# The flags of the search spread from 128 rows instead of 8

## The chip, the core and the metric

The kernel runs on one core of a Trainium2 chip (trn2). The metric is device time in microseconds for one execution of the whole program, the median over several runs. The engines are TensorE (PE in the rows, its weight loads PEld), VectorE (DVE), ScalarE (ACT), GpSimd (POOL) and SyncE (SP, which issues DMAs). They run side by side and wait for each other by semaphores.

## What is computed

Three parts follow each other: a gated linear attention over 4 x 8 heads of 768 steps, an assignment of 3072 tokens to 8 experts with room for exactly 384 tokens each, whose two matrices are then applied, and a gated two-branch layer at the end.

```python
def _moe_ref(x, w_gate, w1, w2):
    cap = N // E                       # 384
    logits = x @ w_gate
    order = np.argsort(-logits.flatten())
    for idx in order:                  # best (token, expert) pair first
        tok, e = int(idx) // E, int(idx) % E
        if assigned[tok] >= 0 or counts[e] >= cap:
            continue
        assigned[tok] = e
        counts[e] += 1
    for e in range(E):
        h = np.maximum(x[assigned == e] @ w1[e], 0.0)
        out[assigned == e] = h @ w2[e]

def _moe2_ref(x, w_a, w_b, w_out):
    return (x @ w_a) * (x @ w_b) @ w_out
```

The greedy order is what makes the assignment hard: which token an expert takes depends on which experts are already full.

## The kernel before

The first stage (attention, the block of lines 167 to 633) leaves the logits in SBUF, token by token on 128 partitions and 24 tiles. The second stage (experts) does the rest in eight turns, one for each expert in the order in which they fill up. It has one instruction stream for each engine, written out by hand; the order within a stream is the order of execution, and semaphores tie the streams together.

**A turn.** TensorE computes, for the 384 tokens of one expert, eight upward tiles (`up`, 8 products of 128x128 by 128x384 each), eight downward tiles (`down`, 9 products), then twelve pairs of the second layer (`pair`, 2 x 8 products into psA and psB) and twelve projections (`project`, 9 products of 320 columns). Each value is split into a high and a low part, which is why there are three products where one would do. In the rows the upward products and the pairs all have line 897, the downward ones line 920, the projections line 947. ACT copies and rounds what comes out, VectorE makes the low parts and the product of a and b (lines 1376, 1380).

**The search.** While turn k runs, the same engines look for the expert that is full next and for its tokens, in the first six turns (a first search, before turn 0, has nothing beside it). A search is a number search in ROUNDS = 11 rounds, each of which fixes one digit. One round is a relay:

1. VectorE, `compare` (line 1156): which keys reach each of 15 or 16 thresholds, into cmp.
2. TensorE, `count` (line 959), three products of the flags with the proposals, into psG; in the first search `count_tiles` (line 967) instead.
3. VectorE, `tally` (lines 1199, 1202), then TensorE, `gather_counts` (line 973), 8 rows by 16 sums into psN16.
4. VectorE, `is_full` (line 1206): for each expert and threshold, is the count at the limit; the answers, 0 or the step of the digit, go to the tile `full` (8 partitions, 15 columns, bfloat16).
5. TensorE, `spread` (line 978): ones times full, so that each of the 128 partitions gets, for each threshold, the sum over the eight experts, into psF.
6. VectorE, `narrow` (line 1214, any_full): the sum becomes the next base; then the next compare.

**Where a round stands in a turn.** For rounds 0 to 5 the spread stands in the middle of an upward tile, behind its third product. Round 6 has no upward tile left and its spread stands alone between `gather_counts` and `down`. Round 7 stands within the psB half of pair 0. Rounds 8, 9 and 10 stand behind projections 0, 1 and 2. Behind projection 3 TensorE does `total` (line 982): the tile of ones, 128 x 128, times mine, 128 x 8, with a wait of its own on VectorE.

GpSimd makes the constant tiles at the end of the first stage (lines 294 to 307), and VectorE waits for all of them at line 613.

Of the kernel before, what the change touches and what calls it, by code (L numbers as in the profile page):

```python
# [7 lines left out]
ALU = mybir.AluOpType  # L8
# [3 lines left out]
F32R = mybir.dt.float32r  # L12
BF16 = mybir.dt.bfloat16
# [3 lines left out]
P = 128  # L17
B, H, S, D = 4, 8, 768, 40
E = 8
DM = H * D  # L20
NT = B * S
CAP = NT // E
# [32 lines left out]
def build(nc, qk, tok, ig, fg, w_gate, w1, w2, w_a, w_b, w_out, out, xs, parts):  # L55
    with ExitStack() as ctx:
        logit = ctx.enter_context(nc.sbuf_tensor("logit", [P, TILES, E], F32))
        identf = ctx.enter_context(nc.sbuf_tensor("identf", [P, P], F32))

        wa = ctx.enter_context(nc.sbuf_tensor("wa", [P, 5, F2], F32R))  # L60
        wb = ctx.enter_context(nc.sbuf_tensor("wb", [P, 5, F2], F32R))
        second = (wa, wb)
        fixed = search_tensors(nc, ctx)
        with ExitStack() as inner:
            attention(nc, inner, logit, identf, qk, tok, ig, fg, w_gate, xs, parts, fixed)
        with ExitStack() as inner:
            experts(nc, inner, logit, identf, second, w_a, w_b, w_out, w1, w2, xs, out, fixed)


def search_tensors(nc, ctx):  # L70
    def sb(name, shape, dt=F32):
        return ctx.enter_context(nc.sbuf_tensor(name, shape, dt))

    return {
        "rown": sb("rown", [P, TILES]), "tilev": sb("tilev", [P, TILES]), "pv": sb("pv", [P, 1]), "digit": sb("digit", [P, 16]),
        "slot": sb("slot", [P, P], BF16), "tie8": sb("tie8", [P, E]), "cols": sb("cols", [P, CAP // P]),
        "ones": sb("ones", [P, P], BF16), "onward": sb("onward", [P, P], BF16),
        "run_on": sb("run_on", [P, TILES]),
        "steps_of": sb("steps_of", [P, len(STEPS), 16]), "start_at": sb("start_at", [P, 3]),
        "sel": sb("sel", [P, TILES]), "was_full": sb("was_full", [P, E]),  # L80
        "own": sb("own", [GI, GJ]), "fold": sb("fold", [GI, 16], F32R),
    }


def attention(nc, ctx, logit, identf, qk, tok, ig, fg, w_gate, xs, parts, fixed):
# [6 lines left out]
    def sem(name):  # L92
        return ctx.enter_context(nc.semaphore(name))
# [68 lines left out]
    sm = {n: sem(n) for n in names}  # L162
# [60 lines left out]
    def _(pool):  # L223
# [77 lines left out]
        pool.memset(fixed["ones"][:, :], 1.0).then_inc(sm["made"], 1)  # L301
        pool.memset(fixed["run_on"][:, :], 1.0).then_inc(sm["made"], 1)
        pool.iota(place_i, [[-16, GJ], [-1, 16]], base=0, channel_multiplier=1).then_inc(sm["made"], 1)
        pool.wait_ge(sm["made"], 10)

        pool.affine_select(out=fixed["onward"][:, :], in_=fixed["ones"][:, :], compare_op=ALU.is_ge, fill=0.0, base=0,
                           pattern=[[-1, P]], channel_multiplier=1).then_inc(sm["made"], 1)
# [168 lines left out]
    def _(dve):  # L476
# [133 lines left out]

        ct = Count(dve, sm["cast_done"])
        also, step = ct.also, ct.step
        dve.wait_ge(sm["made"], 11)
        also(dve.tensor_copy(fixed["rown"][:, :], rowi))
        also(dve.tensor_copy(fixed["tilev"][:, :], tilei))
        also(dve.tensor_copy(fixed["pv"][:, :], pi))
# [19 lines left out]
class Count:  # L636
# [8 lines left out]
    def also(self, ins):  # L645

        self.n += 1
        ins.then_inc(self.sem, 1)
# [11 lines left out]
DIGITS = [(lv, s, i == 0, i == len(digits) - 1) for lv, digits in enumerate(SEARCHES) for i, s in enumerate(digits)]  # L660
# [9 lines left out]
GJ = TILES // NG  # L670
GI = GJ * 16


def experts(nc, ctx, logit, identf, second, w_a, w_b, w_out, w1, w2, xs, out, fixed):
# [8 lines left out]
    def sb(name, shape, dt=F32):  # L683
        return ctx.enter_context(nc.sbuf_tensor(name, shape, dt))
# [4 lines left out]
    def sem(name):  # L689
        return ctx.enter_context(nc.semaphore(name))  # L690
# [41 lines left out]
    rown, tilev, pv, slot, tie8, cols, ones = (fixed[n] for n in """rown tilev pv slot tie8 cols ones""".split())  # L732
    onward, run_on, steps_of, start_at, sel, was_full, own, fold = (fixed[n] for n in """onward run_on steps_of start_at sel was_full own fold""".split())
# [14 lines left out]
    eq = sb("eq", [P, TILES])  # L748
    base = [sb(f"base{n}", [P, 1]) for n in range(2)]
    cmp = sb("cmp", [P, TILES, 16], BF16)  # L750
    full = sb("full", [E, 15], BF16)
    own_cnt = sb("own_cnt", [GI, E, GJ])
    part_cnt = sb("part_cnt", [GI, E], F32R)
    any_full = sb("any_full", [P, 15])
# [31 lines left out]
    psN = psT[:, at:at + 15]  # L786
    psN16 = psT[:, at:at + 16]
    psG = psT[0:GI, 0:GJ * E]
    psF = psT[:, at + 16:at + 31]
# [9 lines left out]
    sm = {n: sem(n) for n in names}  # L799
# [79 lines left out]
    def _(pe):  # L879
# [95 lines left out]
        def spread(p, r):  # L975

            pe.wait_ge(sm["full_ready"], p * ROUNDS + r + 1)
            pe.matmul(psF, ones[0:E, :], full[:, :], start=True, stop=True).then_inc(sm["spread"], 1)  # L978

        def total(p):  # L980
            pe.wait_ge(sm["given_ready"], p + 1)
# [16 lines left out]
        with pe.Fori(0, ROUNDS) as r:  # L998
            count_tiles(r)
            spread(0, r)  # L1000
# [10 lines left out]
        def turn(k, beside):  # L1011
            p = k + 1
            search = beside == "search"
            for f in range(FT):
                if f < FT - 1:
                    up(k, f + 1, (lambda: spread(p, f - 1)) if search and f else None)
                elif search:
                    spread(p, f - 1)
                down(k, f, (lambda: count(p, f)) if search else None)
                if search:  # L1020
                    gather_counts(p, f)
# [125 lines left out]
    def _(dve):  # L1147
# [55 lines left out]

        def is_full(p, r):
            dve.wait_ge(sm["counted"], p * ROUNDS + r + 1)
            dve.tensor_scalar(full[:, :], psN[0:E, :], CAP - 0.5, float(DIGITS[r][1]), ALU.is_ge, ALU.mult
                              ).then_inc(sm["full_ready"], 1)

        def narrow(p, r):
# [129 lines left out]
        start = ct.n  # L1339
        for r in range(ROUNDS):  # L1340
            is_full(0, r)
            narrow(0, r)
# [23 lines left out]
        def turn(k, beside):  # L1366
# [17 lines left out]
            for f in range(FT - 1):  # L1384
                if search and f:
                    narrow(p, f - 1)
                if search:
                    tally(p, f)
                h_low(k, f + 1)
                if search:  # L1390
                    is_full(p, f)
                if early and f in SPLIT_EARLY:
                    low_parts(0, SPLIT_EARLY[f])
                if early and f == WO_EARLY:
                    low_out(0)
# [6 lines left out]
            if search:  # L1402
                is_full(p, FT - 1)
                narrow(p, FT - 1)
# [89 lines left out]
```

## Time and profile before

| | us |
|---|---|
| median of 3 runs | 919.02 |
| lowest and highest run | 914.65, 921.96 |
| profiled execution | 922.04 |
| its span, first to last instruction | 920.3 |
| TensorE matmul busy | 812.3 (88%) |
| VectorE busy | 609.3 (66%) |
| ScalarE busy | 287.1 (31%) |
| GpSimd busy | 169.8 (18%) |

The busy time of TensorE is that of its products with their modelled ends; products follow each other more closely than they last, so the distance from start to start says more than the duration of one. A row of the timeline gives the start, the duration, the engine, the line and the tiles that are written and read; behind it, in brackets, how long the engine was idle before and who released it.

### The profile page before, as it was taken

Reading aid. Unit: us, or ns where it says so; the run is one execution under the profiler, and the core shown is the slowest. Engines: PE = TensorE matmul, PEld = TensorE weight load, DVE = VectorE, ACT = ScalarE, POOL = GpSimd, SP = SyncE. Lnnn points to the kernel's source line nnn. Section 1 sums busy time; section 2 is a strip of 40 time slices with the busy share of each in tenths; the row PEclk is TensorE's granted clock in tenths of the full one; section 3 lists DMA queues with packets and bytes.
Section 4 is the critical chain, followed back from the end, with each engine's and each line's share of the span. In section 5 each row is a group of like instructions: output and inputs, shape, how many; then the busy total and the mean of one; then the engine's idle time right before and its main releaser. Section 6 shows DMA issues by size and latency. Waiting matters only on the chain.

```text
span 920.3 us, 16627 instructions
## 1 busy us (share of the span) xinstructions
PE 812.3 (88%) x5858; PEld 752.0 (82%) x5858; DVE 609.3 (66%) x1756; ACT 287.1 (31%) x538; POOL 169.8 (18%) x195
## 2 busy tenths in 40 slices
PE   1999999322789999999999999999999999999995
PEld 0899999211669988998898889889978999999995
DVE  7778888667557876686668567856876683374221
ACT  4434442211223432252234123412432252243221
POOL 6555665281000110011002001100110011011001
PEclk9999999555789999999999999999999999999998
DMA  4866661603200410130023003200500230050000
GB/s 115 246 190 209 208 207 61 213 0 116 75 22 22 134 37 2 47 102 21 0 63 92 15 0 97 71 0 2 141 25 0 63 84 22 1 137 34 1 1 22
DMA packets 51624, 66.63 MB, mean 72 GB/s; under 512 B 6376, under 2 KB 42232, under 8 KB 51576
## 3 DMA queue, kind: packets, MB, share of 16 engines
q1 hardware_dynamic: 37352, 50.31, 18.0%
q0 software_dynamic: 2368, 7.88, 3.1%
q10 hardware_dynamic: 11856, 7.87, 2.8%
q8 instruction: 22, 0.36, 0.2%
q14 instruction: 26, 0.21, 0.1%
HBM read 57.88 MB, written 8.16 MB: 72 GB/s over the span
## 4 chain that ended last, share of the span: by engine, by line
PE 50%; DVE 23%; issue 3%; ACT 3%; DMA 1%; POOL 1%; SPq 0%; DVEq 0%; ACTq 0%; POOLq 0%
PE psA L897 21%; PE acc L920 11%; PE psB L897 8%; PE acc L947 7%; DVE at_slot L1294 3%; DVE ab L1376 2%; DVE ab_lo L1380 2%; DVE w_lo L1318 2%; ACT ab_hi L1120 2%; DVE cmp L1156 2%; DVE w_lo L1314 2%; PE psT L978 1%; DVE w_hi L1316 1%; PE psT L959 1%; PE psT L967 1%
## 5 line engine op out<-in xcount | busy, mean ns | idle before, releaser
L897 PE MATMUL psA<-x_hi,wa 128*128 128x384 f32 x480 | 136.2, 348 | 0.5 <-DVE x_lo L1401 0.4
L897 PE MATMUL psB<-x_hi,wb 128*128 128x384 f32 x480 | 131.8, 339 | 0.0
L852 POOL DMA_INDIRECT xg<-xs_dram,idx_g x24 | 25.1, 1046 | 468.0 <-DVE idx_g L1308 463.2
L1129 ACT COPY a_sb<-psA 128x384 f32<-128x384 f32 x96 | 46.1, 480 | 174.9 <-PE psB L897 174.9
L897 PE MATMUL psA<-x_lo,wa 128*128 128x384 f32 x288 | 96.8, 336 | 0.0
L897 PE MATMUL psB<-x_lo,wb 128*128 128x384 f32 x288 | 96.5, 335 | 0.0
L947 PE MATMUL acc<-wo_hi,ab_hi 128*128 128x320 f32 x288 | 92.9, 323 | 1.0 <-DVE ab_lo L1380 1.0
L1376 DVE TENSOR_TENSOR ab<-a_sb,psB 128x384 f32<-128x384 f32 x96 | 52.9, 551 | 58.4 <-ACT a_sb L1129 57.4
L947 PE MATMUL acc<-wo_lo,ab_hi 128*128 128x320 f32 x288 | 88.9, 309 | 0.0
L947 PE MATMUL acc<-wo_hi,ab_lo 128*128 128x320 f32 x288 | 88.8, 308 | 0.0
L1380 DVE TENSOR_TENSOR ab_lo<-ab,ab_hi 128x384 fp32r<-128x384 f32 x96 | 53.6, 559 | 52.3 <-ACT ab_hi L1120 48.1
L897 PE MATMUL psA<-x_hi,w_hi 128*128 128x384 f32 x192 | 74.6, 388 | 14.3 <-DVE w_lo L1321 7.5
L897 PEld LDWEIGHTS psA<-x_hi,wa 128*128 128x128 f32 x480 | 83.1, 188 | 4.1 <-DVE x_lo L1401 2.1
L897 PEld LDWEIGHTS psB<-x_hi,wb 128*128 128x128 f32 x480 | 85.9, 188 | 0.1
L1104 ACT ACTIVATE h_hi<-psA 128x384 fp32r<-128x384 f32 x64 | 31.5, 492 | 173.5 <-PE psA L897 168.5
L1120 ACT CAST ab_hi<-ab 128x384 fp32r<-128x384 f32 x96 | 49.2, 513 | 92.2 <-DVE ab L1376 92.2
L920 PE MATMUL acc<-h_hi,w_hi 128*128 128x384 f32 x192 | 71.1, 371 | 0.0
L897 PE MATMUL psA<-x_lo,w_hi 128*128 128x384 f32 x192 | 66.3, 345 | 0.0
L920 PE MATMUL acc<-h_lo,w_hi 128*128 128x384 f32 x192 | 65.9, 343 | 0.0
L920 PE MATMUL acc<-h_hi,w_lo 128*128 128x384 f32 x192 | 65.7, 342 | 0.0
L874 POOL DMA_INDIRECT out_dram<-o_sb,idx_s x24 | 24.1, 1003 | 190.1 <-ACT o_sb L1084 185.2
L947 PEld LDWEIGHTS acc<-wo_hi,ab_hi 128*128 128x128 f32 x288 | 54.1, 188 | 3.9 <-DVE ab_lo L1380 3.1
(236 smaller groups left out, 1742.9 us busy)
## 6 DMA issues: line engine op xcount, KB each, us to landing
w_raw<-in_w_dram SPq DMA_DIRECT2D x32, 320.0 KB, 3.1
w_raw<-in_w_dram SPq DMA_DIRECT2D x32, 256.0 KB, 3.0
toks<-in_tok_dram SPq DMA_DIRECT2D x24, 324.0 KB, 3.6
qks<-in_qk_dram SPq DMA_DIRECT2D x48, 160.0 KB
w_raw<-in_w_dram SPq DMA_DIRECT2D x64, 64.0 KB, 2.8
gate<-in_tok_dram SPq DMA_DIRECT2D x6, 640.0 KB, 5.7
xs_dram<-y ACTq DMA_DIRECT2D x24, 160.0 KB, 3.4
qst<-in_qk_dram ACTq DMA_DIRECT2D x48, 60.0 KB
```

What stands on the lines that cost most here:

```text
L852: pool.indirect_dma_start(out=xg[:, t, 0:DM], out_offset=None, in_=xrows, in_offset=bass.IndirectOffsetOnAxis(ap=idx_g[:, t:t + 1], axis=0 ...
L874: pool.indirect_dma_start(out=out, out_offset=bass.IndirectOffsetOnAxis(ap=idx_s[:, t:t + 1], axis=0), in_=o_sb[:, t, :], in_offset=None). ...
L897: last = pe.matmul(ps, w, x, start=(n == 0), stop=(n == len(steps) - 1))
L920: last = pe.matmul(acc[m][:, 0:CAP], w[q][:, f % FQ, c], x[n][:, :], start=(f == 0 and j == 0), stop=(f == FT - 1 and j == 2))
L947: last = pe.matmul(acc[t][:, 0:DM], x[n][:, c], w[:, g, :], start=(g == 0 and j == 0), stop=(g == GT - 1 and j == 2))
L1104: act.activation(h_hi[f % 2][:, :], psA[f % 2][:, 0:CAP], ACT.Relu).then_inc(sm["h_hi_ready"], 1)
L1120: act.copy(ab_hi[g % 2][:, :], ab[g % 2][:, :]).then_inc(sm["ab_hi_ready"], 1)
L1129: act.copy(a_sb[g % 2][:, :], psA[g % 2][:, 0:CAP]).then_inc(sm["a_copied"], 1)
L1156: dve.scalar_tensor_tensor(out=cmp[:, :, :], in0=key[lv][:, :].unsqueeze(2).broadcast_to([P, TILES, 16]), scalar=start_at[:, lv:lv + 1] if ...
L1294: last = dve.tensor_scalar(at_slot[i][:, j, :], slot[:, :], prow[:, i * ST + j:i * ST + j + 1], None, ALU.is_equal)
L1376: dve.tensor_tensor(ab[g % 2][:, :], a_sb[g % 2][:, :], psB[g % 2][:, 0:CAP], ALU.mult).then_inc(sm["ab_done"], 1)
L1380: dve.tensor_tensor(ab_lo[g % 2][:, :], ab[g % 2][:, :], f32(ab_hi[g % 2][:, :]), ALU.subtract).then_inc(sm["ab_ready"], 1)
```

## The change

The tile `full` gets 128 partitions in place of 8. It moves from the second stage's own tiles to those that live through both stages. GpSimd sets it to zero once, near the end of the first stage, and counts that on the semaphore `made`, whose two waits ask for one more. `is_full` writes the first eight partitions, as before. `spread` now multiplies the whole 128 x 128 tile of ones by all 128 rows of `full`; rows 8 to 127 are zero, so the sums are the same.

```diff
@@ search_tensors
-        "own": sb("own", [GI, GJ]), "fold": sb("fold", [GI, 16], F32R),
+        "full": sb("full", [P, 15], BF16), "own": sb("own", [GI, GJ]), "fold": sb("fold", [GI, 16], F32R),
@@ attention, GpSimd
-        pool.wait_ge(sm["made"], 10)
+        pool.memset(fixed["full"][:, :], 0.0).then_inc(sm["made"], 1)
+        pool.wait_ge(sm["made"], 11)
@@ attention, VectorE
-        dve.wait_ge(sm["made"], 11)
+        dve.wait_ge(sm["made"], 12)
@@ experts
-    full = sb("full", [E, 15], BF16)
+    full = fixed["full"]
@@ experts, TensorE, spread
-            pe.matmul(psF, ones[0:E, :], full[:, :], start=True, stop=True).then_inc(sm["spread"], 1)
+            pe.matmul(psF, ones[:, :], full[:, :], start=True, stop=True).then_inc(sm["spread"], 1)
@@ experts, VectorE, is_full
-            dve.tensor_scalar(full[:, :], psN[0:E, :], CAP - 0.5, float(DIGITS[r][1]), ALU.is_ge, ALU.mult
+            dve.tensor_scalar(full[0:E, :], psN[0:E, :], CAP - 0.5, float(DIGITS[r][1]), ALU.is_ge, ALU.mult
```

On GpSimd, at the end of the first stage, the program before (the names are tiles, the numbers partitions by elements):

```order
L301 MEMSET ones 128x128
L302 MEMSET run_on 128x24
L303 IOTA ints 128x128
L306 AFFINE_SELECT onward<-ones 128x128
L64 UNCONDITIONAL_BRANCH
```

and the changed one:

```order
L301 MEMSET ones 128x128
L302 MEMSET run_on 128x24
L303 IOTA ints 128x128
L304 MEMSET full 128x15
L307 AFFINE_SELECT onward<-ones 128x128
L64 UNCONDITIONAL_BRANCH
```

One memset has come in ahead of the last constant; on TensorE, VectorE, ScalarE and SyncE the instructions and their order are the same, only that `spread` reads 128 rows. The tiles that are allocated behind `full` in its new place all start 32 bytes later in their partitions.

## Rows read from the trace of the kernel before

**Rows 1.** The page: TensorE's granted clock, in tenths, over 40 slices.
```profile
PEclk9999999555789999999999999999999999999998
```

**Rows 2.** Line 978, TensorE's idle time before it: releaser, us, times.
```profile
  issue: 14.2, 60
```

**Rows 3.** The chain of waits: start us, us, what; one turn and the next.
```profile
414.18 1.65 PE psA L897 x8
...
463.68 0.11 PE psT L978
...
471.05 0.49 ACT a_sb L1129
...
500.24 1.65 PE psA L897 x8
```

**Rows 4.** Timeline, TensorE, a spread behind a projection: start us, us, engine, line, operation.
```profile
626.02 0.31 PE L947 MATMUL acc<-wo_hi,ab_lo 128*128 128x320 f32 x1
626.26 0.18 PE L978 MATMUL psT<-full,ones 8*128 8x15 bf16 x1
626.37 0.62 PE L897 MATMUL psA<-x_hi,wa 128*128 128x384 f32 x2
626.82 0.34 PE L897 MATMUL psA<-x_lo,wa 128*128 128x384 f32 x1
```

**Rows 5.** Timeline, TensorE, the total behind projection 3 of the same turn.
```profile
639.86 0.31 PE L947 MATMUL acc<-wo_hi,ab_lo 128*128 128x320 f32 x1
640.01 0.18 PE L982 MATMUL psT<-mine,ones 128*128 128x8 bf16 x1
640.05 0.60 PE L897 MATMUL psA<-x_hi,wa 128*128 128x384 f32 x2
640.48 0.35 PE L897 MATMUL psA<-x_lo,wa 128*128 128x384 f32 x1
```

**Rows 6.** Timeline, TensorE, round 0: the spread in an upward tile, and the count after.
```profile
422.23 0.34 PE L897 MATMUL psA<-x_lo,w_hi 128*128 128x384 f32 x1
422.50 0.18 PE L978 MATMUL psT<-full,ones 8*128 8x15 bf16 x1
422.61 0.44 PE L897 MATMUL psA<-x_hi,w_hi 128*128 128x384 f32 x1
422.89 0.34 PE L897 MATMUL psA<-x_hi,w_lo 128*128 128x384 f32 x1
423.06 0.34 PE L897 MATMUL psA<-x_lo,w_hi 128*128 128x384 f32 x1
...
424.11 0.26 PE L959 MATMUL psT<-ohc,cmp 128*128 128x64 bf16 x3
```

**Rows 7.** Timeline, VectorE, the compares behind the spreads of rounds 0 and 3.
```profile
422.99 0.62 DVE L1156 SCALAR_TENSOR_TENSOR cmp<-key,base,steps_of 128x384 bf16<-128x384 f32 x1
...
434.25 0.62 DVE L1156 SCALAR_TENSOR_TENSOR cmp<-key,start_at,steps_of 128x384 bf16<-128x384 f32 x1
```

**Rows 8.** Timeline, TensorE, the count behind the spread of round 3.
```profile
434.62 0.34 PE L920 MATMUL acc<-h_lo,w_hi 128*128 128x384 f32 x1
434.92 0.26 PE L959 MATMUL psT<-ohc,cmp 128*128 128x64 bf16 x3
```

**Rows 9.** Timeline, TensorE, the count behind the spread of round 6.
```profile
444.90 0.26 PE L959 MATMUL psT<-ohc,cmp 128*128 128x64 bf16 x3 [0.27 <-DVE cmp L1156]
```

**Rows 10.** Timeline, VectorE, first search: reads of a spread's and of the total's result.
```profile
171.89 0.23 DVE L1214 TENSOR_SCALAR_CACHE_REDUCE any_full<-psT,start_at 128x15 f32<-128x15 f32 x1 [0.28 <-PE psT L978]
...
208.83 0.17 DVE L1246 TENSOR_SCALAR now_full<-psT 128x8 f32<-128x8 f32 x1 [0.28 <-PE psT L982]
```

**Rows 11.** Timeline, the end of the first stage: GpSimd's constants, VectorE's first use.
```profile
162.05 0.47 POOL L306 TENSOR_SCALAR_AFFINE_SELECT onward<-ones 128x128 bf16<-128x128 bf16 x1
...
162.88 0.17 DVE L614 CAST rown<-ints 128x24 f32<-128x24 int32 x1
```

**Rows 12.** Line 286: engine, operation, count; duration ns min/median/max, first and last start.
```profile
L286 POOL TENSOR_TENSOR st_old<-state,dec x24: 727/737/744, 25.6 to 156.0; 120x328 f32<-120x328 f32 x24
```

## The prediction

> **What bounds the kernel now.** I read the page first, for the clock: TensorE is granted its higher level, 2.4 GHz, but for the first search and the start of the first turn [rows 1]. The profiled execution took 922.04 us, 1.7 us more than its span of 920.3 and 3.0 us above the median of 919.02. Then the line of the matmul that the change touches, line 978. It runs 7 x 11 = 77 times, 66 of them inside the six turns that carry a search, and before 60 of them TensorE's array stood without a new start for 14.2 us in all, 0.24 us each, with no engine named as the releaser [rows 2]. Then the chain of waits, to see whether TensorE's time counts there. In a steady turn (the same row comes back after 86.06 us) the chain lies on TensorE for most of the way from the first upward product at 414.18 to the end of pair 5 at 471.05, where ACT takes it over, and the last spread, at 463.68, is on it [rows 3]. From there it runs over VectorE (places, one-hot tiles, weight splits) for 29.2 us, until the next turn's first product at 500.24. The spreads all lie in the TensorE part. So a spread that costs less shortens the turn, as long as VectorE's part of the round doesn't come last.
>
> **What a spread costs now.** I read it from start to start in TensorE's timeline. Behind a projection [rows 4]: from the last product of the projection to the spread 0.24, to the next pair 0.11, to its third product 0.45: 0.80 us. The closest thing to the changed spread is already in the program, in the same place behind a later projection: the total of line 982, the same 128x128 tile of ones against 8 columns from all 128 rows, with a semaphore wait of the same kind in front of it [rows 5]: 0.15, 0.04 and 0.43, so 0.62 us. The two differ by 0.18. Without either matmul it would be 0.15 and two times 0.17 (the pitch, below), about 0.50: the spread costs 0.30, the total 0.12. In the middle of an upward product [rows 6]: 0.27, 0.11, 0.28, against a pitch of 0.17 between undisturbed products (422.89 to 423.06), so 0.66 in place of 0.35, a cost of 0.31; with the total's 0.12 in its place the saving is 0.19. What the rows show is a wait of about 0.1 us ahead of the 8-row matmul and another 0.1 behind it, which the 128-row one in the same place doesn't have. That the number of rows is the cause is what I infer: output partitions, stationary tile, type and wait are the same in both.
>
> **Which of the eleven rounds give it back.** Rounds 0, 1, 2, 4 and 5 stand in upward tiles with room behind them: VectorE's compare of round 0 ends at 423.61, the count that needs it starts at 424.11 [rows 6, 7]. They give 5 x 0.19 = 0.95. Round 3 has two more VectorE steps (eq, key), and its successor already waits: the count starts 0.30 after the product in front of it, not 0.17, and cmp ended 0.05 before it [rows 7, 8]. Only the part ahead of the spread counts there, 0.27 - 0.17 = 0.10; the part behind it turns into a longer wait for cmp. Round 6 has no products between its sums and its spread, so the spread starts when VectorE has written full, and the count behind it waits another 0.27 us for cmp [rows 9]: whatever TensorE saves there it waits. So it gives nothing. Round 7, in the psB half of the first pair, stands among products of the same 384 columns as an upward tile's and has a count far behind it: 0.19. Rounds 8, 9 and 10 follow projections: 3 x 0.18 = 0.54. That makes 0.95 + 0.10 + 0 + 0.19 + 0.54 = 1.78 us a turn, times six turns 10.7 us. In the first of them two spreads run at or near 1.2 GHz [rows 1]; I take the same 0.19 for them, since a wait at the lower clock can only be as long or longer in time. The bounds of this sum: from below 6 x 10 x 0.07 = 4.2 us, if only the gap behind the spread goes (0.11 against 0.04) and the wait ahead of it belongs to the semaphore; from above 6 x 11 x 0.31 = 20 us, the whole cost of a spread as if it took nothing. I take the value of the total because its row is the same operation in the same place.
>
> **The other edits.** In the first search every round is a serial relay of TensorE and VectorE. From the end of VectorE's write to its next read of the result the trace shows 0.28 us of idle around the 8-row spread and 0.28 around the total there [rows 10]. So 128 rows cost and save nothing in these eleven: 0, give or take 11 x 0.01. VectorE writes 8 rows of full as before. The memset is one more GpSimd instruction in front of affine_select; a memset of 15 columns can hardly take longer than that affine_select over 128 columns, 0.47 us, which ends at 162.52, while VectorE, whose wait now asks for one more, starts on the constants only at 162.88 [rows 11]. The cover is 0.36 us, so I take 0; at 0.47 it would be 0.11 once. The new place of full moves every tile allocated behind it by its 30 bytes, rounded up; that is a rival below. The sum is -10.7 us: 922.04 gives 911.4 for an execution like the profiled one, and from the median 919.02 it gives 908.3. I predict 908.5.
>
> **What the skill says against it.** The 8-row spread lasts 0.18 us and the 128-row total 0.18 [rows 4, 5], so by durations alone nothing is won. The Trainium skill ("TensorE: Matmul & The Clock Gate", section "Why this matters for your kernels") says that a single matmul with a contraction of 32 takes as long as one with 128, and gains only where several run side by side. By that the sum would be zero and the time 919. The durations agree with it; the starts in the same rows don't, and my sum goes by the starts.
>
> **Rivals.**
> 1. The forecast, chance 0.73.
> 2. Part of it is lost on VectorE (0.11). After a spread VectorE does any_full and cmp and is done 1.11 us after the spread's start, while TensorE has 1.61 us of products before the count [rows 6, 7]. The change takes about 0.09 off TensorE's side, and 0.05 goes from the end of cmp to the count [rows 7, 8]. That leaves 0.3 to 0.4 us, so I expect no wait; if the arrival of cmp mattered in all rounds as in round 3, each of the ten would give 0.10, so 1.0 us a turn, 6 us in all: 913.
> 3. Nothing changes (0.09). The idle time ahead of line 978 would be the price of its wait on a semaphore, with the weights fetched only after it. For it: the profile names no releaser. Against: the total waits too and shows no gap [rows 5]. Time 919.
> 4. Slower (0.03). The 32-byte step moves the operands of the turns (all but wa and wb, which are allocated ahead of it) from a multiple of 64 bytes to an odd multiple of 32. If TensorE read them more slowly there, the place would be each of the 436 large products of a turn; about two thirds of them lie on the chain, 2,300 over eight turns. The gain is gone at 10.7 / 2,300 = 4.6 ns per product, and 1% slower, 928, needs (10.7 + 9.2) / 2,300 = 8.7 ns on a pitch of 0.17 us [rows 6]. Against: in the first stage buffers whose size is an odd multiple of 32 bytes (st_old, 1312 bytes) stand at both kinds of address in turn, and over all of them GpSimd's durations spread by 17 ns in 737 [rows 12]. That is another engine, so it weighs less than it seems.
> 5. More than forecast, 12 to 15 us (0.04), if the waits at the lower clock are dearer or a shorter first turn brings the full clock earlier: 905.
>
> **Range and chances.** The forecast's own range is 906 to 912: 9 to 12 us off a base that itself ran from 914.65 to 921.96. The 80% range takes in most of the partial case and the rival with more: 904 to 914.5; outside it lie no change, slower, and the tails. A change of 1% (9.2 us) is about what a measurement of this kernel can tell from no change, and the forecast stands only 1.5 us beyond it. I give faster by over 1% 0.68 (most of the forecast, and the fifth case), within 1% 0.29 (the rest of the forecast, the partial case and no change), slower 0.03.
>
> **What the changed profile would show.** Line 979 in place of 978, 128 rows, with its idle time by issue gone from 14.2 us to a few; starts of 0.15, 0.04, 0.43 around a spread behind a projection and about 0.17, 0.04, 0.26 in an upward tile; the wait in front of the count of round 3 up from 0.12 to about 0.2; round 6 as before; turns of 84.3 us in place of 86.06; the stretch in which VectorE leads unchanged at 29 us; the first search as long as before. I am wrong if the intervals stay at 0.27 and 0.11 (rival 3), if they shrink but the turn doesn't (rival 2), or if the pitch of 0.17 between products grows (rival 4).

## The result and the profile after

| | before | changed |
|---|---|---|
| median of 11 runs, us | 918.89 | 912.33 |
| lowest and highest run | 914.65, 921.96 | 906.65, 914.73 |
| profiled execution | 922.04 | 909.61 |
| its span | 920.3 | 907.9 |

The ratio of the changed kernel to the one before is 0.9926 (95% interval 0.9905 to 0.9946): 6.8 us less (5.0 to 8.7), where 10.7 were worked out and 908.5 us predicted. The time lies in the 80% range (904 to 914.5), but just above the forecast's own 906 to 912, and the gain is a third short. It is a change of 0.7%; the prediction had given 0.68 to more than 1% and 0.29 to less. The two profiled executions are 12.4 us apart and would hide the missing third, so part of the question is what they leave out.

**The spread.** All of the changed kernel's lines have moved up by one; line 979 is the spread. The view of that line, its idle time and who waited for it:

```profile
L979 PE MATMUL psT<-full,ones x77: 182/183/237, 171.2 to 708.9; 128*128 128x15 bf16 x77
its engine sat idle before it (us, times) until:
  DVE full L1207: 11.8, 34
  issue: 6.8, 42
```

The idle time that no engine was named for has fallen from 14.2 us in 60 places [rows 2] to 6.8 in 42; what is behind VectorE's full stays at 11.8. The timeline of TensorE in the changed kernel, round 0 of the same turn, in an upward tile (start us, us, engine, line, operation):

```profile
415.88 0.33 PE L921 MATMUL acc<-h_lo,w_hi 128*128 128x384 f32 x1
416.05 0.17 PE L974 MATMUL psT<-fold,part_cnt 128*8 128x16 f32 x1
416.08 0.42 PE L898 MATMUL psA<-x_hi,w_hi 128*128 128x384 f32 x1
416.34 0.34 PE L898 MATMUL psA<-x_hi,w_lo 128*128 128x384 f32 x1
416.51 0.34 PE L898 MATMUL psA<-x_lo,w_hi 128*128 128x384 f32 x1
416.69 0.18 PE L979 MATMUL psT<-full,ones 128*128 128x15 bf16 x1
416.73 0.42 PE L898 MATMUL psA<-x_hi,w_hi 128*128 128x384 f32 x1
416.99 0.34 PE L898 MATMUL psA<-x_hi,w_lo 128*128 128x384 f32 x1
```

Around the spread, from start to start, this is 0.18, 0.04 and 0.26 us, against 0.27, 0.11 and 0.28 [rows 6]: 0.18 less. The same view behind a projection, and the total further on:

```profile
446.98 0.31 PE L948 MATMUL acc<-wo_hi,ab_lo 128*128 128x320 f32 x1
447.13 0.18 PE L979 MATMUL psT<-full,ones 128*128 128x15 bf16 x1
447.17 0.59 PE L898 MATMUL psA<-x_hi,wa 128*128 128x384 f32 x2
447.60 0.34 PE L898 MATMUL psA<-x_lo,wa 128*128 128x384 f32 x1
...
460.45 0.18 PE L983 MATMUL psT<-mine,ones 128*128 128x8 bf16 x1
...
544.68 0.18 PE L983 MATMUL psT<-mine,ones 128*128 128x8 bf16 x1
```

0.15, 0.04 and 0.43: the spread now has exactly the intervals of the total [rows 5], where it had 0.24, 0.11 and 0.45 [rows 4]. The last two rows are a turn apart: 84.23 us, and the five such distances of this execution are 84.16 to 84.27, where it was 86.06 [rows 3] (85.94 to 86.06 over all five). That is 1.8 us a turn; the forecast had 1.78.

**The two rounds that were to give less.** The same view at the count of round 3 and around the spread of round 6:

```profile
428.17 0.34 PE L921 MATMUL acc<-h_lo,w_hi 128*128 128x384 f32 x1
428.57 0.26 PE L960 MATMUL psT<-ohc,cmp 128*128 128x64 bf16 x3
...
436.55 0.17 PE L974 MATMUL psT<-fold,part_cnt 128*8 128x16 f32 x1
437.01 0.18 PE L979 MATMUL psT<-full,ones 128*128 128x15 bf16 x1 [0.28 <-DVE full L1207]
437.09 0.44 PE L921 MATMUL acc<-h_hi,w_hi 128*128 128x384 f32 x1
...
438.18 0.26 PE L960 MATMUL psT<-ohc,cmp 128*128 128x64 bf16 x3 [0.31 <-DVE cmp L1157]
```

The count of round 3 starts 0.40 us after the product ahead of it, 0.30 before [rows 8]: 0.10 us of what the spread saved has turned into a wait for cmp. The count of round 6 waits 0.31 us, 0.27 before [rows 9]: what the spread saved there TensorE waits. Both are as forecast.

**What did not move.** VectorE's reads in the first search, changed kernel, timeline:

```profile
171.41 0.23 DVE L1215 TENSOR_SCALAR_CACHE_REDUCE any_full<-psT,start_at 128x15 f32<-128x15 f32 x1 [0.29 <-PE psT L979]
...
208.20 0.17 DVE L1247 TENSOR_SCALAR now_full<-psT 128x8 f32<-128x8 f32 x1 [0.28 <-PE psT L983]
```

0.29 and 0.28 against 0.28 and 0.28 [rows 10]; the search from its first compare to mine took 38.27 us, 38.41 before. The stretch led by VectorE, from the end of pair 5 to the next turn's first product, is the 29.19 us from 463.54 to 492.73, 29.2 before [rows 3]. The constants, where the memset came in:

```profile
161.78 0.13 POOL L304 MEMSET full<- 128x15 bf16 x1
161.98 0.41 POOL L307 TENSOR_SCALAR_AFFINE_SELECT onward<-ones 128x128 bf16<-128x128 bf16 x1
```

They end at 162.39, and VectorE takes up line 615 at 162.76, a cover of 0.37 us, where it was 0.36 [rows 11].

So by the trace each term of the sum was there, in the turns and in the first search. What was missing in the time had to be something that a sum over the turns can't see.

### The profile page after: what moved, and what is told of

It is laid out like the page before. It is cut to its first block, busy times and chain, and to the rows that moved or that the text cites. A ratio compares the mean times of both kernels' runs of the same rounds, so it can differ in the third digit from the quotient of the medians.

```text
span 907.9 us, 16628 instructions
## 1 busy us (share of the span) xinstructions
PE 799.9 (88%) x5858; PEld 746.8 (82%) x5858; DVE 609.9 (67%) x1756; ACT 286.7 (32%) x538; POOL 169.4 (19%) x196
## 4 chain that ended last, share of the span: by engine, by line
PE 47%; DVE 26%; issue 3%; ACT 3%; DMA 1%; POOL 1%; SPq 0%; DVEq 0%; ACTq 0%; POOLq 0%
PE psA L898 18%; PE acc L921 11%; PE psB L898 8%; PE acc L948 6%; DVE at_slot L1295 3%; DVE cmp L1157 3%; DVE ab L1377 3%; DVE w_lo L1319 2%; DVE ab_lo L1381 2%; ACT ab_hi L1121 2%; DVE w_lo L1315 2%; DVE w_hi L1317 1%; PE psT L960 1%; PE psT L968 1%; DVE x_lo L1333 1%
## 5 line engine op out<-in xcount | busy, mean ns | idle before, releaser
L853 POOL DMA_INDIRECT xg<-xs_dram,idx_g x24 | 25.1, 1045 | 455.9 <-DVE idx_g L1309 451.0
L1130 ACT COPY a_sb<-psA 128x384 f32<-128x384 f32 x96 | 46.0, 479 | 169.5 <-PE psB L898 169.5
L1105 ACT ACTIVATE h_hi<-psA 128x384 fp32r<-128x384 f32 x64 | 31.4, 490 | 165.8 <-PE psA L898 160.9
```

The costliest lines, as they stand in the source:

```text
L853: pool.indirect_dma_start(out=xg[:, t, 0:DM], out_offset=None, in_=xrows, in_offset=bass.IndirectOffsetOnAxis(ap=idx_g[:, t:t + 1], axis=0 ...
L1105: act.activation(h_hi[f % 2][:, :], psA[f % 2][:, 0:CAP], ACT.Relu).then_inc(sm["h_hi_ready"], 1)
L1130: act.copy(a_sb[g % 2][:, :], psA[g % 2][:, 0:CAP]).then_inc(sm["a_copied"], 1)
```

## The experiments

All ratios are to the kernel before, timed beside it on the same chip, with the 95% interval.

### Is it the place?

The change does two things that can be taken apart: it gives the spread 128 rows, and it moves the tiles allocated behind full by 32 bytes. These are all of the first stage's own, and the second stage's up to the old place of full; the ones behind that (own_cnt and on) stand where they stood, since full no longer takes its 32 bytes there. The forecast had put the move at nothing. Three kernels: the one before once more, the changed one once more, and the changed one with only its spread undone.

```diff
 place only, against the changed kernel
-            pe.matmul(psF, ones[:, :], full[:, :], start=True, stop=True).then_inc(sm["spread"], 1)
+            pe.matmul(psF, ones[0:E, :], full[0:E, :], start=True, stop=True).then_inc(sm["spread"], 1)
```

> The kernel before, unchanged, as a control. Over 11 runs each, the medians of before and changed differ by 6.6 us, while the two profiled executions differ by 12.4 us: 8.9 us in the five turns that run at full clock throughout (1.8 us each), 3.2 us in the first turn, 0.7 us ahead of it, and 0.4 us given back behind the turns. Theory A (the spreads are worth 1.8 us a turn, everything else scatters with the clock): this kernel's ratio to before is 1.000 within 0.2%, and its second profile shows turns of 86.0 us again, but a first turn, a first stage or a first search that differs from the first profile by 1 to 4 us, with another share of low clock. Theory B (the parts outside the turns repeat exactly and the profiled pair is typical): all parts agree with the first profile within 0.3 us.

> The changed kernel again, for a second profile and a second interval. Theory A: turns of 84.25 us as in the first profile, first turn and the parts ahead of it 1 to 4 us off the first profile; the ratio between 0.987 and 0.993. Theory B: the same profile part by part within 0.3 us, and a ratio near 0.987 (12 us). Theory C (the new places of the tiles cost something in the long stages, so that the spreads' 10.7 us are partly paid back): the ratio stays near 0.993 and the first stage, from the start to the first search, is 1 to 4 us longer than that of the kernel before, again and again.

> The changed kernel with one part undone: the spread reads 8 rows of ones and of full again, while the tile keeps its 128 partitions, its memset and its new place, so all tiles behind it stand 32 bytes further as in the changed kernel. Theory A: ratio 1.000 within 0.3%, turns of 86.05 us, intervals around the spread of 0.27, 0.11, 0.28 in an upward tile and 0.24, 0.11, 0.45 behind a projection. Theory C: 2 to 4 us slower than before (1.003 to 1.005), with the loss outside the turns. If the memset or the place carried the gain: turns of 84.3 us here too.

| | median us | ratio |
|---|---|---|
| before, again | 917.65 | 0.9996 (0.9973 to 1.0019) |
| changed, again | 911.82 | 0.9925 (0.9902 to 0.9948) |
| place only | 923.64 | 1.0055 (1.0036 to 1.0075) |

The place alone costs 5.0 us (0.0055 x 918). From place only to the changed kernel it is 11.8 us, which is what the 128 rows bring where both stand in the same place, against 10.7 in the sum. Place only has turns of 85.90 to 85.97 us, like those of before: its loss is not in the turns, and so not in TensorE's large products, where the prediction had looked for it.

### Which tiles, and which multiple?

The second question has two parts. A padding of 32 bytes behind full moves the later tiles by 64 bytes in all from where they were; if 64 were the multiple that counts, it would win the loss back. And 32 bytes put ahead of different tiles of the kernel before tell in which stage the sensitive ones are.

```diff
 pad64, against the changed kernel
-        "full": sb("full", [P, 15], BF16), "own": sb("own", [GI, GJ]), "fold": sb("fold", [GI, 16], F32R),
+        "full": sb("full", [P, 15], BF16), "pad": sb("pad", [P, 8]), "own": sb("own", [GI, GJ]), ...
 before_pad32, against the kernel before: all tiles behind it
+        "pad": sb("pad", [P, 8]), "own": sb("own", [GI, GJ]), "fold": sb("fold", [GI, 16], F32R),
 pad_attention, against the kernel before: the first stage's own tiles only
+    pad = sb("pad", [P, 8])
 pad_experts, against the kernel before: the second stage's own tiles only
+    pad = sb("pad", [P, 8])
```

> The changed kernel with one unused tile of 32 bytes behind full, so that the tiles behind it stand 64 bytes further than before instead of 32. Theory C (tiles that begin at an odd multiple of 32 bytes make the DMAs of the first stage slower, which costs some 4 to 6 us at its second column of tiles): the loss goes, ratio 0.987 to 0.989, first wait of the second column as in the kernel before. Theory D (what costs is the longer life of the tile, the memset or another order of the runs, and not the address): ratio stays at 0.9925.

> The kernel before with one unused tile of 32 bytes where full stands in the changed one, and nothing else: no memset, no other wait, spread on 8 rows. Theory C: slower by 0.4 to 0.7% like the kernel that had the place, the memset and 8 rows. Theory D: 1.000 within 0.2%.

> The kernel before with the unused 32 bytes ahead of the first stage's own tiles alone; the second stage's tiles keep their places. Theory C: all of the loss is here, 1.004 to 1.007, since the extra wait is at tile 4 of the first stage. If the first search or the weights' loads carry the loss: 1.000 to 1.002.

> The kernel before with the unused 32 bytes ahead of the second stage's own tiles alone. Theory C: 1.000 to 1.002, the most that is possible being the 1 to 1.7 us by which the first search was longer in two of three shifted profiles. If the matmuls' operands carried the loss (the mechanism of the prediction's rival 4): 1.004 to 1.007, with a longer pitch in the turns.

| | median us | ratio |
|---|---|---|
| pad64 | 910.38 | 0.9917 (0.9891 to 0.9943) |
| before_pad32 | 922.56 | 1.0056 (1.0026 to 1.0085) |
| pad_attention | 921.91 | 1.0048 (1.0025 to 1.0071) |
| pad_experts | 918.10 | 1.0000 (0.9977 to 1.0023) |

An unused tile of 32 bytes makes the kernel before as much slower as the whole place did, and it does so through the first stage's tiles; moving the second stage's has no cost that shows (1.0000, give or take 0.0023). That fells the place as the prediction had it, with TensorE's operands of the turns. pad64 did not come back to the expected 0.987 to 0.989, a miss; its interval alone reaches down to 0.9891, but its profile has the same late load as the changed kernel's (below), so 64 doesn't look like the multiple. By the addresses that the program before allocates, twelve tiles of the first stage that DMAs fill start at a multiple of 256 bytes in their partitions: arow, mrow, the four of qks, the four of qst, toks0 and gate. No shift by 32 or 64 keeps that. The other three of toks and the two of y, which are stored from, don't start at one in either kernel. (The expectation of pad256 counts nine.)

### 256 bytes, and how many rows

If 256 is the multiple, 224 bytes of padding behind the 32 of full bring the gain back, and 96 (so that all stands off by 128) don't. Beside them stand two kernels on the other half of the change: a spread over 64 and one over 96 rows, once each.

```diff
 pad256 and pad128, against the changed kernel
-        "full": sb("full", [P, 15], BF16), "own": ...
+        "full": sb("full", [P, 15], BF16), "pad": sb("pad", [P, 56]), "own": ...
+        "full": sb("full", [P, 15], BF16), "pad": sb("pad", [P, 24]), "own": ...
 rows64 and rows96, against the changed kernel
-            pe.matmul(psF, ones[:, :], full[:, :], start=True, stop=True).then_inc(sm["spread"], 1)
+            pe.matmul(psF, ones[0:64, :], full[0:64, :], start=True, stop=True).then_inc(sm["spread"], 1)
+            pe.matmul(psF, ones[0:96, :], full[0:96, :], start=True, stop=True).then_inc(sm["spread"], 1)
```

> The changed kernel with an unused tile of 224 bytes behind full, so that every tile behind stands 256 bytes further. In the kernel before, the nine tiles of the first stage that DMAs fill in rows of 512 bytes and more (arow, mrow, qks, qst, toks0, gate) all begin at a multiple of 256 bytes; a shift of 32 or 64 takes them off it, one of 256 does not. Theory C2 (a DMA into SBUF costs more when its rows begin off a multiple of 256 bytes): ACT's queue back at 2.8% of the span in place of 3.0%, and ratio 0.9870 to 0.9890. Theory E (64 bytes already took part of the loss away, the rest is scatter; the address does not matter further): ratio 0.991 to 0.993.

> The same with 96 unused bytes, a shift of 128. Theory C2: the rows begin 128 bytes off a multiple of 256, so the queue's share stays at 3.0% and the ratio near 0.992. If a multiple of 128 is enough: 2.8%, and a ratio like that of the shift by 256.

> The changed kernel with the spread over 64 rows of ones and full. Theory A1 (what costs is that the matmul uses a part of the array's rows, so that the products around it can't overlap with it): intervals of 0.27, 0.11, 0.28 as with 8 rows, turns of 86.0 us. Theory A2 (the cost falls with the number of rows): intervals between those of 8 and 128 rows, turns near 85.2.

> The changed kernel with the spread over 96 rows. Theory A1: more than 64 rows take the whole array, so the intervals are those of 128 rows, 0.18, 0.04, 0.26, and the turns 84.25 us. Theory A2: a little of the cost is left, turns near 84.7.

pad256 took 908.27 us, ratio 0.9892 (0.9867 to 0.9917), and pad128 911.02 us, 0.9919 (0.9887 to 0.9950). Both came as the multiple of 256 has it, though their intervals overlap, so one more experiment stands below. Not all of the 2.8 us between the two is the first stage: the turns of pad128 are 84.37 to 84.45 us, those of pad256 84.25 to 84.37, which is about 0.5 us over the turns, and unexplained. The single runs were 919.92 us for 64 rows and 913.27 for 96. What they were for is in TensorE's timeline. Over 64 rows:

```profile
420.20 0.34 PE L898 MATMUL psA<-x_lo,w_hi 128*128 128x384 f32 x1
420.47 0.18 PE L979 MATMUL psT<-full,ones 64*128 64x15 bf16 x1
420.58 0.44 PE L898 MATMUL psA<-x_hi,w_hi 128*128 128x384 f32 x1
420.85 0.34 PE L898 MATMUL psA<-x_hi,w_lo 128*128 128x384 f32 x1
```

and over 96:

```profile
420.40 0.34 PE L898 MATMUL psA<-x_lo,w_hi 128*128 128x384 f32 x1
420.58 0.18 PE L979 MATMUL psT<-full,ones 96*128 96x15 bf16 x1
420.62 0.42 PE L898 MATMUL psA<-x_hi,w_hi 128*128 128x384 f32 x1
420.88 0.33 PE L898 MATMUL psA<-x_hi,w_lo 128*128 128x384 f32 x1
```

64 rows have the intervals of 8 (0.27, 0.11, 0.27) and turns of 85.99 to 86.04 us, 96 rows those of 128 (0.18, 0.04, 0.26) and turns of 84.13 to 84.24. It isn't the number of rows as such, then: the cost is there in two sizes, and the step lies between 64 and 96. The gap is the same ahead of the small matmul and behind it, 0.09 and 0.07 us. The Trainium skill ("TensorEngine Tiling (Array Packing)", section "Key Properties") says that a change of the array's tiling mode drains TensorE. The step between 64 and 96 rows would fit that, if 96 rows take the whole array as 128 do. Another row tells against it: gather_counts has all 128 rows but only 8 output columns, so a narrow part of the array would do for it too, and it shows no gap between the same large products (0.17 and 0.03 us around 416.05 in the changed kernel, in the first rows above). What is shown is that few rows cost and few columns don't; that a change of mode is the reason is not shown.

### The spread alone, with nothing moved

The last experiment changes the rows of the spread and no tile's place at all.

```diff
 against the kernel before
@@ experts
-    full = sb("full", [E, 15], BF16)
+    full = sb("full", [P, 15], BF16)
@@ experts, GpSimd, its first instruction
+        pool.memset(full[:, :], 0.0).then_inc(sm["made"], 1)
+        pool.wait_ge(sm["made"], 1)
@@ experts, TensorE and VectorE
-            pe.matmul(psF, ones[0:E, :], full[:, :], start=True, stop=True).then_inc(sm["spread"], 1)
+            pe.matmul(psF, ones[:, :], full[:, :], start=True, stop=True).then_inc(sm["spread"], 1)
-            dve.tensor_scalar(full[:, :], psN[0:E, :], CAP - 0.5, ...
+            dve.tensor_scalar(full[0:E, :], psN[0:E, :], CAP - 0.5, ...
@@ experts, VectorE, ahead of the first search
+        dve.wait_ge(sm["made"], 1)
```

> The spread over 128 rows with every tile where it was: full keeps its 32 bytes among the second stage's tiles (it now has 128 partitions there), GpSimd zeroes it in its first instruction of the second stage, and VectorE waits for that once, ahead of the first search. The address theory (the changed kernel loses about 5 us in the first stage because its DMAs' rows start 32 bytes off a multiple of 256): the first stage is as before, the queue of 11856 packets has 2.8% and that of 37352 packets 18.0%, the turns last 84.2 to 84.3 us as in the changed kernel, from the first turn to the end about 8.5 us less than before, and the first turn 2.5 less: ratio to the kernel before 0.987 to 0.989, as with the 224 bytes of padding. The rival (what the address costs is not in the first stage, or the padding's gain was chance or came from another tile's place): 0.991 to 0.994, as in the changed kernel itself.

It took 907.00 us, ratio 0.9892 (0.9861 to 0.9922), turns of 84.24 to 84.36 us. That is 9.9 us less than before, and the forecast of 908.5 is 1.5 us off it. With pad256 it is the best version here. Its interval alone just reaches the rival's 0.991 to 0.994. Taken together it is clear: each run divided by the median of the kernel before that was timed beside it, the 12 runs of place kept and pad256 have a mean about 2.8 us (1.1 to 4.5) below that of the 29 runs of the four kernels with 128 rows and moved tiles (changed twice, pad64, pad128).

### Where in the first stage the time goes

No timed experiment says this; the 14 profiles do. Two stand here: the kernel before (its second profile) and place only, whose programs differ by the place and the memset. First the page's rows on the DMA queues (packets, megabytes, share of 16 engines' span), the kernel before, again:

```profile
q1 hardware_dynamic: 37352, 50.31, 18.0%
q10 hardware_dynamic: 11856, 7.87, 2.8%
```

place only:

```profile
q1 hardware_dynamic: 37352, 50.31, 18.1%
q10 hardware_dynamic: 11856, 7.87, 3.0%
```

The same packets and bytes take longer. Times the span, q10's packets took 2.8% of 915.3, 25.6 us, and 3.0% of 922.1, 27.7 us. Over the 14 profiles it is 25.3 to 25.8 us in the five whose first-stage tiles stand where they stood or 256 bytes further (before twice, pad_experts, pad256, place kept), and 27.2 to 28.3 in the nine others; q1's are 164.8 to 165.8 against 166.5 to 169.5. The percentages are rounded to 0.1, that is to 0.9 us of a span; added up from the single packets in the traces, q10 has 25.1 to 25.5 against 26.9 to 28.0, and q1 165.1 to 165.8 against 166.1 to 169.5. Neither pair of ranges overlaps.

The packets also say in which form the time is lost. Most are not slower: the median 512-byte packet of qst (on q10) takes 27 ns in all 14 profiles. But a tenth of them take longer than 27 to 29 ns in the five, and longer than 40 to 48 ns in the nine. The 2048-byte packets of qks (on q1) have the same median, 84 ns, and their upper quarter begins at 84 ns in the five and at 89 to 114 in the nine. The stores from y are slower too (mean 56 to 57 ns against 60 to 62), though y stands off a multiple of 256 in all kernels; the loads of toks and gate are not. That looks like packets that hold each other up now and then, and not like a fixed price on each packet of a moved tile.

Then where TensorE feels it. Its weight loads, timeline, at the start of the first stage's second round of row loads, the kernel before, again (in brackets the idle time and its releaser):

```profile
41.80 0.23 PEld L395 LDWEIGHTS psE<-mrow,arow 40*128 40x128 bf16 x8 [0.21 <-DMA mrow<-parts_dram]
```

place only:

```profile
45.48 0.23 PEld L396 LDWEIGHTS psE<-mrow,arow 40*128 40x128 bf16 x8 [3.69 <-DMA mrow<-parts_dram]
```

mrow is a small load (12 KB), issued on SyncE's queue at 37.55 us in the one and 37.74 in the other, behind the large ones. The stretches 20 to 40 and 44 to 52 us by engine (us of busy time, instructions; then TensorE's granted clock, the DMA engines' share, GB/s), the kernel before, again:

```profile
20.00:40.00 20.00, 19.43 (x183) 18.33 (x184) 12.58 (x24) 5.70 (x7) 11.26 (x13) 1.00 0.78 231
44.00:52.00 8.00, 8.00 (x85) 7.70 (x86) 6.14 (x15) 1.59 (x3) 4.89 (x6) 1.00 0.76 229
```

place only:

```profile
20.00:40.00 20.00, 19.13 (x181) 18.02 (x182) 12.48 (x23) 5.81 (x8) 11.41 (x13) 1.00 0.79 219
44.00:52.00 8.00, 6.51 (x50) 6.32 (x52) 2.54 (x6) 1.41 (x2) 3.16 (x4) 0.79 0.43 141
```

At nearly the same busy share the DMA engines moved 219 GB/s in place of 231. The row load behind that backlog comes 3.7 us later, TensorE stands for 3.7 us, and its granted clock over the following stretch is 0.79 of 2.4 GHz instead of all of it, which makes the wait dearer than it is long. VectorE's fourth and fifth use of psS show the sum, the kernel before, again, timeline:

```profile
42.24 1.21 DVE L581 TENSOR_TENSOR prob<-psS,decay 128x1024 f32<-128x1024 f32 x1
48.28 1.23 DVE L581 TENSOR_TENSOR prob<-psS,decay 128x1024 f32<-128x1024 f32 x1 [0.17 <-issue]
```

place only:

```profile
42.50 1.21 DVE L582 TENSOR_TENSOR prob<-psS,decay 128x1024 f32<-128x1024 f32 x1
53.09 1.23 DVE L582 TENSOR_TENSOR prob<-psS,decay 128x1024 f32<-128x1024 f32 x1 [0.17 <-issue]
```

This step takes 6.04 us and 10.59. Over the profiles it is 6.04 to 8.77, mean 6.7, in the five with the old alignment, and 6.25 to 11.54, mean 9.8, in the nine without; the wait for mrow has a mean of 0.7 and 2.7 us, the rate from 20 to 40 us one of 229 and 221 GB/s (223 to 231 and 214 to 227). The step behind it has a mean of 5.5 and 5.8 us. The first is 5.8 to 6.9 us long in both groups, and all others 5.2 to 6.3. So the loss is felt at one late load: 3.1 us in its step and 0.3 in the next, of the 3.7 us by which the first search starts later on average.

It also explains the two profiles that were compared first. The same weight load and the same stretch in the first profile of the kernel before, timeline and stretches:

```profile
43.49 0.23 PEld L395 LDWEIGHTS psE<-mrow,arow 40*128 40x128 bf16 x8 [2.12 <-DMA mrow<-parts_dram]
...
44.00:52.00 8.00, 8.00 (x70) 7.79 (x70) 3.51 (x9) 1.77 (x3) 3.33 (x4) 0.79 0.40 119
```

and in the changed kernel's:

```profile
43.42 0.23 PEld L396 LDWEIGHTS psE<-mrow,arow 40*128 40x128 bf16 x8 [1.38 <-DMA mrow<-parts_dram]
...
44.00:52.00 8.00, 8.00 (x71) 7.79 (x71) 4.46 (x10) 1.87 (x4) 3.35 (x4) 0.81 0.47 139
```

The kernel before happened to be profiled with a late load, a clock of 0.79 and a step of 8.77 us, the changed one with much the same and 8.42: the pair showed the whole gain and none of the loss. The chip's arrival times vary from execution to execution; the alignment shifts how often the load is late: the step is above 8 us in one profile of the five and in eight of the nine.

The Trainium skill ("DMA: Bandwidth & Descriptors", section "How a descriptor splits into AXI transactions") has a rule with the same multiple: the transactions of a DMA descriptor start at multiples of 256 bytes, and a descriptor that starts off one costs additional beats (32 bytes each) for bytes that are read and not used. The traces agree in part. Off by 32, 64 and 128 bytes all cost (26.9 to 28.0 us of q10's packets), and the move by 256 did not. But the rule speaks of what is read, and these loads write the moved tiles; and a cost on every descriptor is not seen in the median packet, 27 ns in all of them.

## Why the prediction came out as it did

**The reading from start to start: right.** That an 8-row matmul costs 0.18 to 0.19 us more than a 128-row one of the same duration was taken from one pair of rows, spread and total, and rested on the number of rows being the cause; the runs with 64 and 96 rows show that it is, with a step between them. The changed kernel has 0.18, 0.04, 0.26 in an upward tile and 0.15, 0.04, 0.43 behind a projection. Rival 3, that the gap belongs to the semaphore's wait, is out: wait and place are unchanged, and rows96 lost the gap while rows64 kept it.

**Which rounds give it back: right.** The sum over the eleven rounds had 1.78 us a turn, and five distances show 1.80. That it came within 0.02 is partly luck, since its terms were read to 0.01 us and there are ten of them. Rounds 3 and 6 went as worked out. Rival 2 is out: VectorE takes nothing from the other rounds. The first turn can only be seen through its own variation: from its first upward product to its total the seven profiles with spreads of 8 or 64 rows have 66.1 us on average (64.2 to 67.4), the seven with 96 or 128 rows 64.4 (62.3 to 65.6); the difference of 1.7 is that of any other turn.

**The first search and the memset at nothing: right.** The reads wait as before, and the cover over the memset is 0.37 us, 0.36 before.

**The step that failed: the new place of full, taken as nothing in the sum.** It costs 5.0 us alone in the kernel before (1.0055; the padding of before_pad32 gives 1.0056, that of pad_attention 1.0048), and 3.0 us in the changed one (from 0.9892 to 0.9925); with intervals of 2 to 3 us on each these agree. The sum's -10.7 with the 5.0 of place only gives -5.7 us, inside the interval of the measured gain (5.0 to 8.7). The 912.33 us lie next to the 913 of rival 2, but that is coincidence: what rival 2 has VectorE take from every round was not there. The prediction had seen that the place was a risk, in its rival 4, and asked there only who reads such tiles inside the turns, that is TensorE. By the rows of that stage its mechanism is excluded as the cause: the turns of place only are as long as before, and over all the kernels with 96 or 128 rows they differ by 0.4 us at most (84.07 to 84.45). Not asked was who else uses an address: the DMAs of the first stage. The engine that was looked up for evidence, GpSimd in line 286 [rows 12], takes 736 ns there in place only, 737 before: it is one that shows no change.

**What could have been seen.** That the first stage was open to slower transfers was in the trace of before: TensorE waits once for a DMA in the first stage, for 2.12 us at 43.49, and behind it the granted clock is 0.79 (the rows above). A transfer that already ends a wait on the critical engine has no cover, so anything that may make transfers slower has to be priced there first.

**What stays open.** Which of the moved buffers matters isn't told apart: the slow packets are those of qks, qst and y, but no kernel moved one of these alone. Why more packets are slow when the tiles stand off a multiple of 256 bytes is open too. That these packets are what makes the load of mrow late is inferred from their coming together in the same nine profiles, not shown by itself. The late load and the step behind it explain 3.4 us on average over single executions, and the timed runs say 3 to 5; whether something else adds the rest these intervals can't tell. That the gap of the 8-row matmul is a change of tiling mode has the step between 64 and 96 rows for it and gather_counts against it.

## What to carry to other kernels

Cost a small instruction by the distances between the starts around it, not by its duration, and look for a neighbour of the same form in the same place that lacks the property in question; here one pair of rows gave the gain per turn. A change that adds or moves a tile is two changes: list who uses the addresses that shift, DMAs included, and let those keep their place relative to 256 bytes, or put the new tile last. And compare two profiles only for what differs by more than two profiles of one kernel do: here a late load that the kernel before had by chance in its profile hid a loss of 3 us.

## What the runs showed of the hardware

- A matmul of 8 or 64 rows among ones of 128 costs about 0.18 us more than one of 96 or 128 rows, half ahead of it (0.27 us from start to start in place of 0.18) and half behind, with the same duration (179 ns at 64 rows, 183 at 128). One of 8 output columns and 128 rows shows no gap (0.17 and 0.03).
- Moving the first stage's tiles in SBUF, DMA buffers among them, by 32, 64 or 128 bytes off a multiple of 256 made the packets of one queue take 26.9 to 28.0 us of 16 engines' time in place of 25.1 to 25.5, and the kernel 3 to 5 us longer; by 256 bytes, nothing. The median packet stayed the same (27 ns for 512 bytes), the slowest tenth began at 40 to 48 ns in place of 27 to 29.
- At the load of mrow a wait of TensorE of 3.7 us was followed by a mean granted clock of 0.79 over the stretch from 44 to 52 us (2.4 GHz in one part of it and 1.2 in the other), and so were five others of 1.4 to 3.9 us (0.79 or 0.81); waits of 2.6, 2.9 and 3.9 us in three more profiles (rows96, changed again, pad64) were followed by 0.57; after waits of 0.2, 1.1 (pad256) and 1.2 us (pad128) the clock stayed at 2.4 GHz.
